# Attention, MoE and gated layer in one kernel: fixed turns of the experts, tile 0's tokens from a short list of its own, high parts first, layer two's lists behind expert 1's weights

## Chip and metric

The kernel runs as one program on one core of a Trainium2 chip. The metric is the device time of one execution in microseconds (us); lower is better. The profile is one such execution, recorded by the hardware profiler. Engines: TensorE (PE; PEld is its weight load), VectorE (DVE), ScalarE (ACT), GpSimd (POOL), SyncE (SP), which here only issues DMAs.

## What is computed

Three stages follow each other. Inputs are float32: q, k, v of shape 2x8x768x64, 16 centroids for each head, 8 experts of 512x1024 and 1024x512, and three matrices of a last layer with 1536 columns.

```python
mask = q_assign[:, :, :, None] == k_assign[:, :, None, :]      # nearest centroid of each query and key
scores = np.where(mask, scale * q @ k.T, -1e9)
attn_out = softmax(scores) @ v                                   # -> x: 1536 tokens x 512

logits = x @ w_gate                                              # 8 experts
expert_idx = np.argmax(logits, axis=1)
for e in range(E):
    mask = expert_idx == e
    out[mask] = gate_w[mask, None] * (np.maximum(x[mask] @ w1[e], 0.0) @ w2[e])

result = ((out @ w_a) * (out @ w_b)) @ w_out
```

For the inputs used, the experts have 198, 119, 169, 188, 162, 192, 206 and 302 tokens, which is 2, 1, 2, 2, 2, 2, 2 and 3 tiles of 128 rows.

## The kernel before

The order of work on each engine is written out by hand; engines wait for each other by semaphores alone (`wait_ge`). On VectorE `link` makes a step wait for the one before it.

**Attention.** 16 heads (`G`), in pairs, six query tiles each. The last step of a head scales its rows of x (`scale_x`, L948) and its share of the gate logits; SP stores the rows to `x_rows` in DRAM (`store_rows`, L444), and POOL adds the logits (`add_logits`, L567), for the last head too. Beside it POOL splits expert 0's weights.

**Weights.** A product of float32 values is made of high and low parts: high x high, high x low and low x high (`product3`, L1291 to L1293, in this order for each slice of the contraction). The weights of an expert are 8 chunks of 128x1024 (`HELD`), 4 for `w1` and 4 for `w2` (`C1`). SP loads chunk `i` into one of 4 stage buffers once chunk `i - 4` is converted (`load_chunk`, L453); POOL converts expert 0's and VectorE all others: `make_high` (L368, a cast) and `make_low` (L372, a subtraction, which raises `s_cv`). Two experts' weights fit in `w_split`. So an expert's chunks overwrite those of the expert two turns earlier, once that expert's last tile is through (`s_hid` for `w1`, `s_yps` for `w2`).

**Routing** (L990 to L1079). From the logits VectorE makes a one-hot of each token's expert (`e_hot`); TensorE multiplies it by a triangle and by ones for each token's rank within its expert, then for the experts' counts, and raises `s_rank` after both. VectorE finds the first tile of each expert (`e_start`), each token's slot, and one-hots of slot row (`row_hot`, one compare of 128x1536) and slot tile. TensorE multiplies them to turn the list round: which token is in each slot (`token_i`, L1032, raises `s_token`). POOL gathers the rows of tiles 0 and 1 by this list (`gather_x`, L620). VectorE then gives a turn to each expert that has tokens (`turn_i`, `turn_start_i`, `turn_expert_i`, raising `s_turns`, L1050), and SP waits for that before it loads the second turn's weights (L506). The last layer's lists (`c_start` to `place_values`, L1056 to L1079) follow at once: 128-row tiles of tokens sorted by expert, without padding. Only then come the conversions of turn 1 (`for r in range(1, E)`).

**Tiles.** `TILES` = 19 tiles of 128 slots. For each, TensorE transposes the gathered rows (`transpose_x`, L1304), makes the hidden layer in two halves of 12 matmuls (`hidden`), transposes it (`transpose_h`, L1328) and makes the output in two halves of 12 matmuls (`expert_out`). `tile(j)` interleaves tile `j` with the hidden halves of tile `j + 1`. ScalarE copies each transposed tile twice, as high part and raw, and POOL subtracts one from the other for the low part (`xT_low` L633, `hT_low` L639). `hidden` of a tile waits for 4 chunks of its expert in `s_cv` and for both parts of x. Where nothing useful is to be done, TensorE multiplies the identity by itself (`spin`, L1144). `find_places` (L1346) is 12 small matmuls for the last layer's lists and stands behind tile 0.

**Last layer.** 36 units of 36 matmuls and their outputs, untouched here.

## Time and profile before

| | |
|---|---|
| median of 3 runs | 841.16 us (841.05 to 843.97) |
| the profiled execution | 842.13 us, its span 839.5 us |
| mean granted TensorE clock | 0.991 |
| PE busy | 814.5 us (97%) |
| DVE busy | 460.5 us (55%) |
| ACT busy | 352.4 us (42%) |
| POOL busy | 363.5 us (43%) |
| DMA | 86.67 MB, mean 103 GB/s |

The profiled execution's time is 2.6 us more than its span, which is the time around it. The chain that ended last lies on PE for 84% of the span, on DVE for 7% and on POOL for 4%. A busy PE counts stand-in matmuls too, and matmuls overlap a little, so that their summed durations say less than the distance of their starts. In a timeline a row gives the start in us, the duration in us, the engine, the line, the operation, what it writes and reads, and in square brackets how long the engine was idle before it and what it waited for.

### The profile page before, as it was taken

What the parts mean: (1) busy time and instruction counts of PE and PEld (TensorE: products, weight loads), DVE (VectorE), ACT (ScalarE), POOL (GpSimd) and SP (SyncE); (2) the same over time, 40 slices, a digit from 0 to 9 for tenths busy, and PEclk for the clock granted to TensorE, in tenths of its full rate; (3) what the DMA queues carried; (4) which work ended last, traced back from release to release, by engine and by line L of the source; (5) the groups of instructions that cost most, each with busy time, mean ns of one, the idle gap of its engine ahead of it and who ended that gap; (6) DMA issues with size and microseconds to landing.
All of it is one profiled execution on the core that took longest, in us unless ns stands there. A gap on an engine that the chain in (4) does not pass through costs nothing.

```text
span 839.5 us, 13318 instructions
## 1 busy us (share of the span) xinstructions
PE 814.5 (97%) x4402; PEld 682.1 (81%) x4403; DVE 460.5 (55%) x705; ACT 352.4 (42%) x711; POOL 363.5 (43%) x295
## 2 busy tenths in 40 slices
PE   8999999999999898999999999999999999999995
PEld 4888898898898487888888888788888888888884
DVE  2879879879886899997777401642121112111110
ACT  1867778778786142434334444211212122121111
POOL 6998988988983344464446454000001000010001
PEclk8999999999999999999999999999999999999998
DMA  7454444454320368776668511500001000010001
GB/s 184 123 124 120 127 129 120 120 132 122 78 84 19 112 223 267 230 263 208 215 204 269 159 38 51 159 16 13 26 13 50 1 13 13 0 51 1 1 0 50
DMA packets 50137, 86.67 MB, mean 103 GB/s; under 512 B 19312, under 2 KB 21360, under 8 KB 50096
## 3 DMA queue, kind: packets, MB, share of 16 engines
q1 hardware_dynamic: 43920, 69.88, 28.6%
q0 software_dynamic: 3440, 11.27, 4.3%
q10 hardware_dynamic: 2736, 4.98, 1.6%
q8 instruction: 25, 0.41, 0.2%
q14 instruction: 16, 0.13, 0.0%
HBM read 73.27 MB, written 11.27 MB: 101 GB/s over the span
## 4 chain that ended last, share of the span: by engine, by line
PE 84%; DVE 7%; POOL 4%; issue 2%; DMA 1%; SPq 0%; ACT 0%; DVEq 0%; POOLq 0%
PE bank L1291 19%; PE bank L1293 19%; PE bank L1292 19%; PE bank L1199 6%; PE bank L1215 4%; PE bank L1183 3%; PE bank L1189 3%; PE bank L1217 3%; DVE w_split L372 2%; PE bank L1228 2%; PE bank L1328 2%; PE bank L1163 2%; DVE w_split L368 2%; PE bank L1214 1%; PE bank L1304 1%
## 5 line engine op out<-in xcount | busy, mean ns | idle before, releaser
L1130 DVE TENSOR_TENSOR ab_raw<-bank,a_sb 128x512 f32<-128x512 f32 x36 | 24.9, 691 | 191.4 <-PE bank L1293 191.4
L958 DVE TENSOR_REDUCE neg_max<-bank 128x1 f32<-128x768 f32 x96 | 91.7, 955 | 37.9 <-PE bank L1189 37.2
L368 DVE CAST w_split<-stage 128x1024 fp32r<-128x1024 f32 x72 | 66.8, 927 | 74.9 <-PE bank L1293 74.4
L372 DVE TENSOR_TENSOR w_split<-stage,w_split 128x1024 fp32r<-128x1024 f32 x72 | 104.6, 1452 | 2.5
L718 ACT ACTIVATE pT_hi<-bank 128x384 fp32r<-128x384 f32 x192 | 84.9, 490 | 46.3 <-PE bank L1199 45.0
L929 DVE TENSOR_TENSOR pT_lo<-bank,pT_hi 128x384 fp32r<-128x384 f32 x192 | 97.5, 550 | 4.5 <-ACT pT_hi L718 4.5
L639 POOL TENSOR_TENSOR hT_lo<-hT_raw,hT_hi 128x512 fp32r<-128x512 f32 x38 | 56.0, 1473 | 89.4 <-ACT hT_raw L777 89.2
L739 ACT ACTIVATE probs<-bank,neg_max 128x768 f32<-128x768 f32 x96 | 87.1, 907 | 11.3 <-DVE neg_max L958 11.3
L1199 PE MATMUL bank<-ident,probs 128*128 128x128 f32 x576 | 81.0, 275 | 1.8 <-ACT probs L739 1.1
L837 ACT ACTIVATE a_sb<-bank 128x512 f32<-128x512 f32 x36 | 21.5, 598 | 136.1 <-PE bank L1293 136.1
L1293 PE MATMUL bank<-x2T_a,w_split 128*128 128x512 f32 x192 | 74.7, 389 | 0.0
L1291 PE MATMUL bank<-x2T_a,w_split 128*128 128x512 f32 x192 | 74.7, 389 | 0.0
L1292 PE MATMUL bank<-x2T_a,w_split 128*128 128x512 f32 x192 | 74.7, 389 | 0.0
L1199 PEld LDWEIGHTS bank<-ident,probs 128*128 128x128 f32 x576 | 65.8, 140 | 10.4 <-DVE pT_lo L929 2.5
L650 POOL DMA_INDIRECT x<-sorted_y,back_i x12 | 11.7, 978 | 129.8 <-PE bank L1340 128.6
L1291 PE MATMUL bank<-w_split,xT_hi 128*128 x152 | 61.7, 406 | 3.5 <-DVE w_split L372 2.6
L1291 PE MATMUL bank<-w_split,hT_hi 128*128 x152 | 63.0, 414 | 0.5 <-issue 0.5
L1215 PE MATMUL bank<-pT_lo,v_split 128*64 128x384 f32 x192 | 61.6, 348 | 0.0
L1293 PE MATMUL bank<-w_split,xT_lo 128*128 x152 | 60.3, 396 | 0.0
L1292 PE MATMUL bank<-w_split,xT_hi 128*128 x152 | 59.9, 394 | 0.0
L1293 PE MATMUL bank<-w_split,hT_lo 128*128 x152 | 59.6, 392 | 0.0
L1292 PE MATMUL bank<-w_split,hT_hi 128*128 x152 | 59.5, 391 | 0.0
(224 smaller groups left out, 1826.0 us busy)
## 6 DMA issues: line engine op xcount, KB each, us to landing
stage<-w SPq DMA_DIRECT2D x64, 512.0 KB, 4.2
q_raw<-qT SPq DMA_DIRECT2D x32, 192.0 KB, 3.7
k_raw<-kT SPq DMA_DIRECT2D x32, 192.0 KB, 3.9
sorted_y<-y_sb ACTq DMA_DIRECT2D x19, 256.0 KB, 4.0
q_pair<-qT SPq DMA_DIRECT2D x8, 384.0 KB, 4.3
k_pair<-kT SPq DMA_DIRECT2D x8, 384.0 KB, 4.9
v_raw<-v_keys SPq DMA_DIRECT2D x16, 192.0 KB, 4.2
stage<-w_a SPq DMA_DIRECT2D x6, 512.0 KB, 4.4
```

What stands on the lines that cost most here:

```text
L368: eng.tensor_copy(dst[:, 0], src).then_inc(s_cvh, 1)
L372: eng.tensor_tensor(dst[:, 1], stage[:, i % STAGES], dst[:, 0].bitcast(F32), ALU.subtract).then_inc(s_cv, 1)
L639: pool.tensor_tensor(hT_lo[:, cols], hT_raw[:, cols], hT_hi[:, cols].bitcast(F32), ALU.subtract).then_inc(s_hl, 1)
L718: act.activation(pT_hi[:, half, part * GT:(part + 1) * GT, j * P:(j + 1) * P], pT_ps[part].rearrange("p (k q) -> p k q", q=P), ACT.Copy).t ...
L739: act.activation(probs[:, qt % 2], scores[qt % 2][:, 0:S], ACT.Exp, bias=neg_max[:, qt % 2:qt % 2 + 1], accum_out=row_sum[:, slot, qt, 0:1 ...
L929: dve.tensor_tensor(pT_lo[dst], pT_ps[part].rearrange("p (k q) -> p k q", q=P), pT_hi[dst].bitcast(F32), ALU.subtract).then_inc(s_pl, 1)
L958: dve.tensor_reduce(neg_max[:, qt % 2:qt % 2 + 1], scores[qt % 2][:, 0:S], AX_X, ALU.max, negate=True).then_inc(s_max, 1)
L1199: last = pe.transpose(pT_ps[part][:, j * P:(j + 1) * P], probs[:, slot, kt * P:(kt + 1) * P], ident[:, :])
L1215: pe.matmul(oT_ps[0:D], v_split[:, slot, kt, 0], pT_lo[:, half, kt], start=False, stop=False)
L1291: pe.matmul(ps, lh, rh, start=first, stop=False)
L1292: pe.matmul(ps, lh, rl, start=False, stop=False)
L1293: return pe.matmul(ps, ll, rh, start=False, stop=last)
```

## The change

1. *Fixed turns.* Each expert has at least one tile: the thresholds that count its tiles begin at -1 (`tile_thr`), and expert `e` has turn `e`. The turn lists go; SP no longer waits for them or reads them. It issues expert 1's first four loads between the last stores of attention and all others behind them.
2. *Tile 0's own short list.* The rank counts from 1. `first_key` is the rank of expert 0's tokens and 0 for all others; 12 compares of 128x128 make its one-hots (`lane_hot`, used again later), and 12 small matmuls give the tokens of tile 0 alone (`first_i`). POOL gathers tile 0 by it and the other tiles by `token_i`. The counts have a PSUM bank and a semaphore of their own, so that this chain waits only for the ranks. `find_slots` moves behind tile 0's first hidden half.
3. *One-hots in pieces.* `row_hot` and the later `lane_hot` are 12 compares of 128x128 against a per-partition scalar in place of one of 128x1536. The row of an expert's first slot comes straight out of one sum.
4. *Logits.* VectorE adds the last head's share itself, and the difference for the softmax comes behind `e_hot`. The gate's sum and reciprocal come behind `token_i`.
5. *High parts first.* In `hidden` and `expert_out` the 8 matmuls with the high part of the left side come first; the wait for the low part stands before the last 4.
6. *Tile 0 and 1 in another order.* Only tile 0 is transposed before the first hidden half; both of its halves are transposed, then comes its output, and tile 1 behind that.
7. *Layer two's lists* stand behind the 8 conversions of expert 1, ahead of expert 2's; `find_places` stands behind tile 1.

The core of the diff (constants of POOL, ScalarE's matching order and semaphores are left out):

```diff
@@ SP @@
-            for c in range(PAIRS - 1, HELD):
-                load_first(c)
+            load_first(HELD - 1)
             store_head(G - 3, 1)
+            load_expert(HELD)
+            load_expert(HELD + 1)
             store_head(G - 2, 0)
+            load_expert(HELD + 2)
+            load_expert(HELD + 3)
             store_rows(G - 1, 1, 0, GT, 2 * G - 1)
             store_rows(G - 1, 1, GT, QT, 2 * G)
-            sp.wait_ge(s_turns, 1)
-            for r in range(1, E):
-                e = sp.value_load(turn_expert_i[0:1, r:r + 1], min_val=0, max_val=E - 1)
...
+            for i in range(HELD + 4, EXPERT_CHUNKS):
+                load_expert(i)
@@ POOL @@
+                token = first_i[:, 0:1] if j == 0 else token_i[:, j:j + 1]
...
-            pool.wait_ge(s_token, 1)
+            pool.wait_ge(s_first, 1)
             gather_x(0, 0)
-            gather_x(1, 1)
...
             xT_low(0, 0)
+            pool.wait_ge(s_token, 1)
+            gather_x(1, 1)
             gather_x(2, 0)
+            hT_low(0, 0)
+            hT_low(0, 1)
             xT_low(1, 1)
             gather_x(3, 1)
-            hT_low(0, 0)
@@ VectorE @@
+            dve.wait_ge(s_rank, 1)
+            link(dve.tensor_tensor(first_key[:, :], rank[:, :, 0], e_hot[:, :, 0], ALU.mult))
+            for t in range(T):
+                dve.tensor_scalar(lane_hot[:, t, :], row_no[:, 0, :], first_key[:, t:t + 1], -1.0,
+                                  ALU.subtract, ALU.is_equal).then_inc(s_fhot, 1)
+            dve.wait_ge(s_counts, 1)
+            link(dve.tensor_tensor(r_et, counts.unsqueeze(2).to_broadcast([P, E, T]), tile_thr[:, :, :], ALU.is_gt))
+            link(dve.tensor_copy(counts_f[:, :], counts))
+            dve.wait_ge(s_firstT, 1)
+            link(dve.tensor_scalar(first_f[:, :], first_token[:, 0:1], float(P), None, ALU.mult))
+            dve.tensor_tensor(first_i[:, :], first_token[:, 1:2], first_f[:, :], ALU.add).then_inc(s_first, 1)
...
+            for t in range(T):
+                dve.tensor_scalar(row_hot[:, t, :], row_no[:, 0, :], slot_lane[:, t:t + 1], None, ALU.is_equal).then_inc(s_thot, 1)
...
+                if r == 1:
+                    make_place_one_hots()
@@ TensorE @@
+            last.then_inc(s_counts, 1)
             for t in range(T):
-                last = pe.matmul(slot_token, row_hot[:, t, :], tile_tokens[:, t], start=(t == 0), stop=(t == T - 1))
-            last.then_inc(s_slotT, 1)
-            spin(20)
+                pe.wait_ge(s_fhot, t + 1)
+                last = pe.matmul(first_token, lane_hot[:, t, :], packed[:, t, 0:2], start=(t == 0), stop=(t == T - 1))
+            last.then_inc(s_firstT, 1)
+            spin(19)
...
+                for c in range(C1):
+                    for part in range(2):
+                        pe.matmul(h_ps[half], xT_hi[:, par, cols(c)], ring((r % 2) * HELD + c, part)[:, cols(half, 512)],
+                                  start=(c == 0 and part == 0), stop=False)
+                if half == 0:
                     pe.wait_ge(s_xl, j + 1)
...
-            pe.wait_ge(s_turns, 1)
             transpose_x(0, 0)
             spin(3)
-            transpose_x(1, 1)
-            spin(3)
-            r_first = turn_of(0)
-            hidden(0, 0, 0, r_first)
-            hidden(0, 0, 1, r_first)
+            hidden(0, 0, 0, 0)
+            find_slots()
+            hidden(0, 0, 1, 0)
             transpose_h(0, 0)
+            transpose_h(0, 1)
+            pe.wait_ge(s_tiles, 1)
...
+                if static(j) and j == 0:
+                    expert_out(0, 0, 0)
+                    transpose_x(1, 1)
+                    expert_out(0, 1, 0)
+                    r_next = expert_of(1)
+                    hidden(1, 1, 0, r_next)
+                    transpose_x(2, 0)
+                    hidden(1, 1, 1, r_next)
+                    transpose_h(1, 0)
+                    return
...
-                if static(j) and j == 0:
+                if static(j) and j == 1:
                     find_places()
```

What that does to the order of instructions shows best on two engines. On VectorE, around the first conversions, the order before is this (`place_hot` and `packed` belong to layer two's lists, L368 and L372 convert a chunk):

```order
L1047 CAST turn_start_i<-turn_start_f 128x8
L1050 CAST turn_expert_i<-turn_expert_f 128x8
L1056 TENSOR_TENSOR r_tmp<-bank,before_e 128x64
...
L1064 TENSOR_TENSOR lane_hot<-row_no,place_lane 128x1536
L1066 TENSOR_TENSOR place_hot<-tile_row,place_tile 128x144
...
L1079 TENSOR_TENSOR place_values<-place_hot,packed 128x1008
L368 CAST w_split<-stage 128x1024
L372 TENSOR_TENSOR w_split<-stage,w_split 128x1024
L368 CAST w_split<-stage 128x1024
```

And this is it in the changed kernel, from the gate's reciprocal to the first conversion of expert 2 (L372 and L376 convert a chunk there; the dots stand for six more of the eight chunks and for the lists' middle):

```order
L1067 TENSOR_TENSOR token_i<-bank,token_f 128x19
L1071 RECIPROCAL gate<-l_sum 128x12
L372 CAST w_split<-stage 128x1024
L376 TENSOR_TENSOR w_split<-stage,w_split 128x1024
...
L1076 TENSOR_TENSOR r_tmp<-counts_f,before_e 128x64
...
L1088 TENSOR_SCALAR lane_hot<-row_no,place_lane_f 128x128 x12
...
L1096 TENSOR_TENSOR place_values<-place_hot,packed 128x1008
L1105 TENSOR_LOAD e_start_i
...
L372 CAST w_split<-stage 128x1024
L376 TENSOR_TENSOR w_split<-stage,w_split 128x1024
```

The lists stood ahead of all conversions and now stand between expert 1's eight and expert 2's.

On TensorE, from the counts to the first tile, before:

```order
L1279 MATMUL bank<-e_hot,ones 128x8 x12
L1144 MATMUL bank<-ident_bf 128x512 x23
L1284 MATMUL bank<-tile_tokens,row_hot 128x38 x12
L1144 MATMUL bank<-ident_bf 128x512 x20
L1304 MATMUL bank<-ident,x_in 128x128 x4
L1144 MATMUL bank<-ident_bf 128x512 x3
L1304 MATMUL bank<-ident,x_in 128x128 x4
L1144 MATMUL bank<-ident_bf 128x512 x3
```

And in the changed kernel, where L1302 is tile 0's short list and L1309 is `find_slots`:

```order
L1298 MATMUL bank<-e_hot,ones 128x8 x12
L1302 MATMUL bank<-packed,lane_hot 128x2 x12
L1162 MATMUL bank<-ident_bf 128x512 x19
L1327 MATMUL bank<-ident,x_in 128x128 x4
L1162 MATMUL bank<-ident_bf 128x512 x3
L1342 MATMUL bank<-w_split,xT_hi 128x512 x8
L1347 MATMUL bank<-w_split,xT_lo 128x512 x4
L1309 MATMUL bank<-tile_tokens,row_hot 128x38 x12
L1342 MATMUL bank<-w_split,xT_hi 128x512 x8
L1347 MATMUL bank<-w_split,xT_lo 128x512 x4
L1354 MATMUL bank<-ident,h_relu 128x128 x8
```

The 12 small matmuls on all slots moved from before the first transposes to behind the first 12 hidden matmuls, and 27 of the 49 stand-in matmuls are gone.

## Rows read from the trace of the kernel before

**Rows 1.** The page: busy time of the engines; one kind of DMA issue.

```profile
PE 814.5 (97%) x4402; PEld 682.1 (81%) x4403; DVE 460.5 (55%) x705; ACT 352.4 (42%) x711; POOL 363.5 (43%) x295
...
stage<-w SPq DMA_DIRECT2D x64, 512.0 KB, 4.2
```

**Rows 2.** Windows: length; busy us of PE, PEld, DVE, ACT, POOL; PEclk, DMA, GB/s.

```profile
272.50:291.20 18.70, 15.30 (x104) 7.20 (x102) 15.92 (x53) 2.30 (x5) 4.54 (x5) 1.00 0.26 83
291.20:322.60 31.40, 31.40 (x160) 25.54 (x160) 30.85 (x32) 11.51 (x22) 18.14 (x12) 1.00 0.73 241
...
330.20:830.00 499.80, 497.74 (x2306) 411.50 (x2305) 190.51 (x206) 143.13 (x255) 112.85 (x87) 1.00 0.27 87
```

**Rows 3.** Timeline of TensorE before tile 3.

```profile
309.54 0.63 PE L1346 MATMUL bank<-place_values,lane_hot 128*128 128x84 bf16 x12
...
322.24 0.39 PE L1293 MATMUL bank<-w_split,hT_lo 128*128 x1
...
325.19 0.49 PE L1291 MATMUL bank<-w_split,xT_hi 128*128 x1 [2.56 <-DVE w_split L372]
```

**Rows 4.** Timeline of VectorE's conversions, and one POOL row beside them.

```profile
294.92 0.69 DVE L368 CAST w_split<-stage 128x1024 fp32r<-128x1024 f32 x1
...
298.58 1.30 POOL L639 TENSOR_TENSOR hT_lo<-hT_raw,hT_hi 128x512 fp32r<-128x512 f32 x1 [4.20 <-ACT hT_raw L777]
...
298.64 1.79 DVE L368 CAST w_split<-stage 128x1024 fp32r<-128x1024 f32 x1
...
312.10 0.69 DVE L368 CAST w_split<-stage 128x1024 fp32r<-128x1024 f32 x1
...
313.96 0.69 DVE L368 CAST w_split<-stage 128x1024 fp32r<-128x1024 f32 x1
...
323.55 1.23 DVE L372 TENSOR_TENSOR w_split<-stage,w_split 128x1024 fp32r<-128x1024 f32 x1
```

**Rows 5.** Timeline of the routing and of tile 0's start, several engines.

```profile
273.30 0.25 DVE L999 TENSOR_REDUCE l_max<-logits 128x12 f32<-128x96 f32 x1 [0.40 <-POOL logits L567]
...
275.39 0.44 PE L1279 MATMUL bank<-e_hot,ones 128*128 128x8 bf16 x12
...
275.94 0.26 DVE L1013 TENSOR_TENSOR r_tmp<-bank,tile_thr 128x96 f32<-128x96 f32 x1 [0.42 <-PE bank L1279]
...
282.25 0.18 DVE L1032 TENSOR_TENSOR token_i<-bank,token_f 128x19 int32<-128x19 f32 x1
...
287.04 0.63 PE L1304 MATMUL bank<-ident,x_in 128*128 128x128 f32 x4 [0.71 <-DMA x_in<-x_rows,token_i]
...
288.88 1.96 POOL L633 TENSOR_TENSOR xT_lo<-xT_raw,xT_hi 128x512 fp32r<-128x512 f32 x1 [3.15 <-ACT xT_raw L767]
```

**Rows 6.** Timeline of VectorE: small instructions that follow each other.

```profile
332.15 0.16 DVE L1098 TENSOR_SCALAR scaled<-bank 128x12 f32<-128x12 f32 x1
332.23 0.16 DVE L1099 TENSOR_SCALAR scaled<-bank 128x12 f32<-128x12 f32 x1
```

**Rows 7.** Timeline of TensorE in the second pair of heads.

```profile
47.41 0.61 PE L1183 MATMUL bank<-k_hl,q_hh 128*128 128x512 f32 x2 [1.25 <-POOL k_hl L548]
```

**Rows 8.** Timeline of VectorE: the lists for layer two.

```profile
286.06 0.23 DVE L1056 TENSOR_TENSOR r_tmp<-bank,before_e 128x64 f32<-128x64 f32 x1
...
287.95 1.75 DVE L1064 TENSOR_TENSOR lane_hot<-row_no,place_lane 128x1536 bf16<-128x1536 bf16 x1
...
289.74 1.26 DVE L1066 TENSOR_TENSOR place_hot<-tile_row,place_tile 128x144 f32<-128x144 f32 x1
...
291.71 1.61 DVE L1076 CAST packed<-gate_rest 128x12 bf16<-128x12 f32 x1
```

**Rows 9.** Windows of TensorE alone: length, busy us (count), PEclk, DMA, GB/s.

```profile
326.20:329.50 3.30, 3.30 (x10) 0.52 0.85 286
8.70:15.30 6.60, 6.60 (x26) 0.52 1.01 191
```

More of the change, by code:

```diff
@@ L338, in attention_moe_gate @@
         UNITS = 3 * FB
[L339 removed]
+        Y_TILES = [min(TILES, ((4 * g + 4) * P - 1 + (E - 1) * P) // P + 1) for g in range(3)]
         EARLY = Y_TILES[0] + 1
@@ L979, in pair @@
                 head(pp, 1)
+            dve.memset(first_f[:, :], 0.0).then_inc(s_hid, 1)
+            dve.memset(first_key[:, :], 0.0).then_inc(s_yps, 1)
             dve.memset(row_sum[:, :, :, 1:2], 1e-9).then_inc(s_line, 1)
@@ L997, in _ @@
             r_tiles = r_tmp[:, 0:TILES * (E - 1)].rearrange("p (j e) -> p j e", e=E - 1)
-            dve.wait_ge(s_logit, G)
+            one_t = lambda m: m[:, :].unsqueeze(2)
+            one_value = lambda i: packed[:, :, i:i + 1]
+            last_b = slice((B - 1) * QT, B * QT)
+            dve.wait_ge(s_logit, G - 1)
+            dve.wait_ge(s_x, 2 * G)
+            link(dve.tensor_tensor(logits[:, last_b, :], logits[:, last_b, :], x_head[:, (G - 1) % 2, :, D:XW], ALU.add))
             link(dve.tensor_reduce(l_max[:, :], logits[:, :, :], AX_X, ALU.max))
-            dve.tensor_tensor(l_dif[:, :, :], logits[:, :, :], by_t(l_max[:, :]), ALU.subtract).then_inc(s_gx, 1)
             link(dve.tensor_tensor(l_eq[:, :, :], logits[:, :, :], by_t(l_max[:, :]), ALU.is_equal))
@@ L1005, in _ @@
+            link(dve.tensor_reduce(tile_e_f[:, :], r_tiles, AX_X, ALU.add))
+            dve.tensor_copy(tile_e_i[:, :], tile_e_f[:, :]).then_inc(s_tiles, 1)
+            dve.wait_ge(s_slotT, 1)
+            link(dve.tensor_scalar(token_f[:, :], slot_token[:, 0], float(P), None, ALU.mult))
+            dve.tensor_tensor(token_i[:, :], slot_token[:, 1], token_f[:, :], ALU.add).then_inc(s_token, 1)
             dve.wait_ge(s_ge, 1)
@@ L1275, in _, with find_slots @@
             for t in range(T - 1):
-                pe.matmul(rank[:, t + 1:T, :], ones[:, :], e_hot[:, t:t + 1, :].to_broadcast([P, T - 1 - t, E]),
-                          start=False, stop=(t == T - 2))
+                last = pe.matmul(rank[:, t + 1:T, :], ones[:, :], e_hot[:, t:t + 1, :].to_broadcast([P, T - 1 - t, E]),
+                                 start=False, stop=(t == T - 2))
+            last.then_inc(s_rank, 1)
             for t in range(T):
                 last = pe.matmul(counts, ones[:, :], e_hot[:, t, :], start=(t == 0), stop=(t == T - 1))
-            last.then_inc(s_rank, 1)
-            spin(23)
-            pe.wait_ge(s_thot, 3)
+            last.then_inc(s_counts, 1)
             for t in range(T):
-                last = pe.matmul(slot_token, row_hot[:, t, :], tile_tokens[:, t], start=(t == 0), stop=(t == T - 1))
-            last.then_inc(s_slotT, 1)
-            spin(20)
+                pe.wait_ge(s_fhot, t + 1)
+                last = pe.matmul(first_token, lane_hot[:, t, :], packed[:, t, 0:2], start=(t == 0), stop=(t == T - 1))
+            last.then_inc(s_firstT, 1)
+            spin(19)
+            def find_slots():
+                pe.wait_ge(s_thot, T + 2)
+                for t in range(T):
+                    last = pe.matmul(slot_token, row_hot[:, t, :], tile_tokens[:, t], start=(t == 0), stop=(t == T - 1))
+                last.then_inc(s_slotT, 1)
             def product3(ps, left, right, first, last):
```

217 lines of the change are left out of this document (101 added, 116 removed).

## The prediction

> **What bounds the kernel now.** I read the page first: TensorE is busy 97% of the span, no other engine more than 55% [rows 1]. So time can only come from TensorE's gaps, its stand-in matmuls on the identity (`spin`), or its clock. The windows by stage show where these lie [rows 2]: after attention (until 272.5 us) 18.7 us of routing with few useful matmuls, 31.4 us without a gap, then a gap and a slow stretch, and from 330.2 on 499.8 us with 497.7 busy at full clock. The change touches the routing, the first two tiles and the gap. The rest can gain nothing: its matmuls, their number and their shapes stay.
>
> The gap has one releaser: the first hidden matmul at 325.19 waits for VectorE's `w_split` (L372) [rows 3]. In the order of TensorE it is tile 3, the first of expert 2. It waits for `s_cv` at 20, the 20th chunk converted; 8 of these are expert 0's, so VectorE must convert 12 chunks after the routing. It starts them at 294.92 and ends the twelfth at 323.55 + 1.23 = 324.78; TensorE follows 0.41 later [rows 3, 4]. VectorE never waits in that stretch (30.85 of 31.4 us busy [rows 2]), so not the weights' DMA but VectorE itself is the limit. **The end of the kernel therefore hangs on when VectorE has done its twelfth chunk, and not on when TensorE starts tile 0.** A chunk takes 1.86 us where nothing disturbs it (CASTs at 312.10 and 313.96 [rows 4]). Twelve are 22.3; from 294.92 to 324.78 are 29.9. The missing 7.5 us are seven stretched instructions, one for each of the seven POOL subtractions in the stretch; the first pair stands at 298.58 and 298.64, a CAST of 1.79 for 0.69 [rows 4]. That is 1.08 us each.
>
> **The first tile's tokens.** First the ends of the chain, then what comes between. The last logits addition moves from POOL to VectorE, where `l_max` waits 0.40 for it [rows 5]; the addition takes most of that itself: 0.1 us saved. `l_dif` leaves the path to `e_hot`: 0.2, what such an instruction of 96 elements takes (0.26 [rows 5]) less its overlap. `first_key` waits for the ranks and no longer for the 12 count matmuls: 0.3 (0.44 from the first start to the last end [rows 5]). So it starts at 275.94 - 0.6 = 275.3 and takes 0.2. Then come 12 compares of 128x128. No such row exists. Independent instructions of 12 elements start 0.08 apart (332.15, 332.23 [rows 6]); a CAST of 1024 takes 0.69 [rows 4] against 0.16 for 12 [rows 6], 0.52 ns an element, which makes 0.15 for 128. Bounds 1.0 and 1.8 us for 12; I take the middle, 1.4. The compare and copy of the counts (0.29 + 0.2) and the two instructions that make `first_i` (0.4) end at 277.8. Today `token_i` ends at 282.25 + 0.18 = 282.43 [rows 5]: **the gather of tile 0 starts 4.6 us earlier**, and its transposes at 287.04 - 4.6 = 282.4 [rows 5]. SP's last stores of `x_rows` are issued when they are today, right after the last x_head; no row shows them late, and I take them as landed.
>
> The VectorE: DVE Perf Modes page of the Trainium skill (section on the TRN2 errata: SBUF-source operations) puts such a bf16 compare from SBUF at 58 + 128/4 cycles, 0.09 us, so 12 at 1.1 us. That is an estimate from the page, inside my bounds; it would take 0.3 from this term and 0.3 from the lists below.
>
> **Tile 0 on TensorE.** High parts first: the first eight matmuls start when `xT_hi` is there, some 1.4 after the transposes, and end at 285.6. The subtraction of the low part starts 1.84 after the transposes, as at 288.88, and takes 1.3 as at 298.58 [rows 4, 5]: ready at 285.8 with the hop between engines. Four more matmuls at 0.23 (322.24 to the end at 322.47 [rows 3]) and the 12 small ones of `find_slots` (some 0.4, as the 12 of the counts [rows 5]) end at 287.3. The second half, the transposes, the output and tile 1's hidden halves follow with small gaps (for the relu, 0.6, and for `hT_lo`), since nothing is interleaved now. I add 60 matmuls at 0.227, five groups of transposes at 0.36 and for the gaps 1.3: the state that today is reached at 309.54, where `find_places` starts [rows 3], is reached at 304.0. With a tile and `find_places`, 12.9 us (309.54 to 322.47), TensorE stands before tile 3 at 316.9, **5.6 us earlier than today**.
>
> **VectorE, the path that counts.** `find_slots` now stands behind tile 0's first hidden half, so VectorE, done with its own routing at about 283.3 (17 chained instructions of 0.2 to 0.4 and 12 compares, 5.5 us, behind 277.8), waits until 287.3 for it. `token_f`, `token_i` and the three instructions of the gate follow, with their chain 1.0 us: 288.3. POOL gets a memset, two small iotas and a select more, and `turn_no`'s iota less, ahead of the k_hl for which TensorE waits 1.25 us at 47.41 [rows 7]. I put that at 0.2 us (0 to 0.5), and it shifts everything. VectorE starts chunk 8 at 288.5 instead of 294.92: 6.4 earlier. Its data is there, since four loads are issued before the end of attention. Each later load has the conversion of three other chunks, 5.6 us, to land in, and takes 4.2 [rows 1].
>
> But the lists for layer two no longer lie ahead of these chunks. They lie between the eighth and the ninth, and tile 3 needs twelve: they are still on the path, only in another place of it. Today they last from 286.06 to 294.92 [rows 4, 8], 8.86 us. Two of them are stretched by POOL, 1.26 for about 0.3 and 1.61 for 0.2 [rows 8]: 6.5 without. The one compare of 1.75 becomes 12 (1.4), one small cast is added (0.2), two fillings of `packed` go (0.2): 6.1. POOL's subtractions in the stretch are eight: the two halves of tile 0, x and both halves of tile 1, x of tiles 2 and 3, and the first half of tile 2. The sum: 288.5 + 22.3 + 6.1 + 8 x 1.08 = 325.5, and TensorE 0.4 later, **325.9 against 325.19: +0.7**. What TensorE gained turns into a gap of 9.0 us in place of 2.6.
>
> Here a rule speaks against the change. The stretched rows show that a POOL subtraction costs VectorE 1.08 us [rows 4]. The SBUF — State Buffer page of the Trainium skill (section "SBUF: two separate sides") says that the pair of ports which both engines share is an exclusive lock for a whole instruction. By it each subtraction would cost up to its own length, 1.3, which is another 1.8 us over eight. The trace agrees with the kind of wait and falls short of that length.
>
> **The clock.** After today's gap the granted clock is full for 1 us and then at 0.52 from 326.2 to 329.5, in the main the 1.2 GHz level [rows 9]: 1.65 us lost. The other stretch at that level lasts 6.6 us, after the thin start of the program [rows 9]: 3.3 lost. I take it that a gap of 9.0 costs no less than today's and no more than that, and choose 2.2, nearer to today's, since only the gap's length differs: +0.5.
>
> **The sum.** 842.13 (the profiled execution) + 0.7 + 0.5 = 843.3. Against the median of the runs, 841.16, that is **842.4 us**. Work costed at nothing: the weight loads (covered by conversions; uncovered, 4 us once), the removed turn instructions (282.35 to 286.06 on VectorE; they fall into the wait for `find_slots` anyway), `find_places` one tile later (in the gap).
>
> **Rivals.**
> 1. *TensorE keeps its lead.* If VectorE were ready by 316.9, the gap and the slow clock would vanish: 5.6 + 2.6 + 1.6 = 9.8 less, 831.4. For it: the first four chunks are loaded early. Against it: VectorE's work up to the twelfth chunk does not fit. It would need the lists off the path and few disturbed instructions; lists at half price (3.0) and half the stretches (4.3) give 7.3, 835, and it would take both. Chance 0.12.
> 2. *The clock falls in tile 0.* Between the last `spin` and the first hidden matmuls lie gaps of some 1.0 and 0.5 us. Today's (0.71 before the transposes [rows 5] and others) leave the clock at 1.00 [rows 2]. If it falls before `find_slots`, 12 matmuls at 0.43 for 0.227 and the transposes make 2.7 us, VectorE waits for them, and the twelfth chunk is late by that; with the full 3.3 at the gap, 842.4 + 2.7 + 1.1 = 846.2, slower by 0.6%. It decides from some nine matmuls at the low level on (1.9 us). Chance 0.10.
> 3. *The change does half of what it says:* POOL disturbs less, since the 24 short compares need few ports or its subtractions meet VectorE waiting. Three stretches fewer and 0.8 for the compares give 838.4. Chance 0.15.
>
> The forecast keeps 0.63.
>
> **How the numbers follow.** Down: 0.8 (compares at 1.0), three stretches (3.2): 838.4. Up: 0.8 (compares at 1.8), 1.8 (the longer stretches), 1.1 (clock): 846.1. The range 838.3 to 846.1 leaves out rival 1 and the end of rival 2. A measurement of this kernel tells 0.5%, 4.2 us, from no change. Faster by more needs less than 837.0: rival 1, 0.12. Slower by more is over 845.4: rival 2 and some of the upper end, 0.10. The rest, 0.78, is no change.
>
> **What would show it.** Right: `first_i` near 277.8; the transposes of tile 0 near 282.4; VectorE's first CAST near 288.5; the twelfth chunk near 325.5; a gap before the first hidden matmul of tile 3 of 7 to 10 us with VectorE as releaser and the clock at half behind it. Wrong: a gap of under 4 us (rival 1), a clock below 1 before 290 us (rival 2), fewer than six stretched instructions (rival 3), or a gap elsewhere, which nothing here foresees.

## The result, and the profile after

The changed kernel takes 846.91 us, the median of 6 runs (846.63 to 848.53), beside 842.5 us for the kernel before on the same chip (841.05 to 844.81): ratio 1.0053, 95% interval 1.0033 to 1.0073. It is slower by 0.5%, 4.5 us above the 842.4 forecast and 0.8 above the range. (The forecast was built on 841.16, the median of the first three of the six times of the kernel before.) The profiled execution took 846.94 us with a span of 845.2.

The page of the changed kernel, for [rows 1]: the engines' busy time, and the loads of weights.

```profile
PE 816.7 (97%) x4387; PEld 685.8 (81%) x4388; DVE 459.2 (54%) x736; ACT 352.8 (42%) x711; POOL 360.6 (43%) x297
...
stage<-w SPq DMA_DIRECT2D x64, 512.0 KB, 4.3
```

This tells no more than that TensorE is still the busy one. The last x_head, with which both kernels enter the part that was changed, is a good mark to divide the span at. It starts at 272.52 before and at 276.00 now, so **3.5 us of the 5.7 by which the span grew lie ahead of the part whose time the prediction added up**, in attention. The windows of TensorE there in the kernel before (stretch, length, busy us, clock, DMA share, GB/s):

```profile
8.00:15.00 7.00, 7.00 (x30) 0.57 1.01 196
15.00:19.50 4.50, 3.88 (x21) 0.92 0.61 193
19.50:35.50 16.00, 14.18 (x97) 1.00 0.54 134
```

And in the changed kernel:

```profile
8.00:15.00 7.00, 5.86 (x44) 1.00 1.03 196
15.00:19.50 4.50, 2.10 (x10) 1.00 0.60 208
19.50:35.50 16.00, 15.91 (x72) 0.57 0.53 132
```

Before, the clock is low from 8 to 15 us, under stand-ins. They take longer, TensorE reaches its wait for POOL's `k_hl` late and idles 0.93 us, and the clock stays full behind it. Now it is full from 8 to 15, the stand-ins end early, TensorE idles 2.49 us, and over the next 16 us the granted clock averages 0.57, under attention's own matmuls: 72 of them in the window instead of 97. The first matmul behind the wait starts at 19.80 before and 19.59 now, so the change to POOL's constants did not move it. Here `k_hl` is what the first scores read; POOL makes it. The row in the timeline of the changed kernel:

```profile
19.59 0.59 PE L1201 MATMUL bank<-k_hl,q_hh 128*128 128x512 f32 x2 [2.49 <-POOL k_hl L554]
```

From x_head on, for [rows 2]: windows of the changed kernel, with the same columns (length; busy us of PE, PEld, DVE, ACT, POOL; PEclk, DMA, GB/s).

```profile
276.00:292.58 16.58, 16.02 (x101) 9.02 (x100) 11.53 (x59) 1.97 (x4) 2.81 (x3) 0.90 0.08 22
292.58:320.76 28.18, 27.93 (x136) 22.25 (x134) 27.49 (x45) 11.65 (x22) 18.23 (x13) 1.00 0.63 206
320.76:335.50 14.74, 6.34 (x27) 4.94 (x27) 14.46 (x17) 0.78 (x2) 0.00 (x0) 0.65 0.58 185
335.50:835.00 499.50, 497.43 (x2305) 411.15 (x2305) 189.60 (x205) 143.05 (x255) 111.13 (x86) 1.00 0.27 87
```

First the routing, then somewhat over two tiles' work without a gap, then a gap and a slow stretch, and the long rest at full clock. The third window is what the forecast called the gap of 9 us; VectorE is busy all through it. The timeline of TensorE there, for [rows 3]:

```profile
319.68 1.08 PE L1417 MATMUL bank<-w_split,hT_lo 128*128 x4
322.10 0.64 PE L1372 MATMUL bank<-place_values,lane_hot 128*128 128x84 bf16 x12 [1.34 <-DVE place_values L1096]
329.80 3.77 PE L1342 MATMUL bank<-w_split,xT_hi 128*128 x8 [7.07 <-DVE w_split L376]
```

TensorE waits 1.34 us for the lists, does `find_places`, and waits 7.07 us for VectorE's twelfth chunk. That makes 9.0 us from 320.76 to tile 3, the length that the forecast gave the gap. Eight matmuls at the low clock then take 3.77. Tile 3 starts 53.80 us after x_head, and 52.67 before. VectorE's timeline of the changed kernel, for [rows 4] and [rows 8]: conversions and lists.

```profile
292.58 0.70 DVE L372 CAST w_split<-stage 128x1024 fp32r<-128x1024 f32 x1
...
296.32 1.79 DVE L372 CAST w_split<-stage 128x1024 fp32r<-128x1024 f32 x1
298.14 2.19 DVE L376 TENSOR_TENSOR w_split<-stage,w_split 128x1024 fp32r<-128x1024 f32 x1
...
306.81 1.78 DVE L372 CAST w_split<-stage 128x1024 fp32r<-128x1024 f32 x1
309.77 1.78 DVE L372 CAST w_split<-stage 128x1024 fp32r<-128x1024 f32 x1
312.73 0.22 DVE L1076 TENSOR_TENSOR r_tmp<-counts_f,before_e 128x64 f32<-128x64 f32 x1
...
313.53 0.71 DVE L1079 TENSOR_TENSOR r_tmp<-r_tmp,e_hot 128x96 f32<-128x96 f32 x1
...
315.49 3.08 DVE L1088 TENSOR_SCALAR lane_hot<-row_no,place_lane_f 128x128 bf16<-128x128 bf16 x12
...
319.30 1.27 DVE L1094 TENSOR_TENSOR gate_rest<-gate_rest,packed 128x12 f32<-128x12 f32 x1
...
320.83 1.21 DVE L1096 TENSOR_TENSOR place_values<-place_hot,packed 128x1008 bf16<-128x1008 bf16 x1
321.96 0.69 DVE L372 CAST w_split<-stage 128x1024 fp32r<-128x1024 f32 x1
```

And the routing, for [rows 5]:

```profile
278.82 0.17 DVE L1034 TENSOR_TENSOR first_key<-bank,e_hot 128x12 f32<-128x12 f32 x1 [0.51 <-PE bank L1294]
279.03 2.04 DVE L1036 TENSOR_SCALAR lane_hot<-row_no,first_key 128x128 bf16<-128x128 bf16 x12
279.34 1.98 PE L1302 MATMUL bank<-packed,lane_hot 128*128 128x2 bf16 x12 [0.25 <-DVE lane_hot L1036]
281.18 5.79 PE L1162 MATMUL bank<-ident_bf 128*128 128x512 bf16 x19
281.67 0.16 DVE L1043 TENSOR_TENSOR first_i<-bank,first_f 128x1 int32<-128x1 f32 x1
286.81 0.60 PE L1327 MATMUL bank<-ident,x_in 128*128 128x128 f32 x4
291.53 0.18 DVE L1066 TENSOR_SCALAR token_f<-bank 128x19 f32<-128x19 f32 x1 [3.58 <-PE bank L1309]
```

The 5.7 us of span are therefore 3.5 ahead of x_head, 1.1 (53.80 - 52.67) from there to tile 3, and 1.1 behind it. The last of these is the clock: it is low until 335.5, which is 5.7 us of work at half speed, 2.8 lost, where 1.65 were lost before [rows 9].

### The profile page after: what moved, and what is told of

Read it like the earlier page. It is cut to its first block, busy times and chain, and to the rows that moved or that the text cites. A ratio compares the mean times of both kernels' runs of the same rounds, so it can differ in the third digit from the quotient of the medians.

```text
span 845.2 us, 13127 instructions
## 1 busy us (share of the span) xinstructions
PE 816.7 (97%) x4387; PEld 685.8 (81%) x4388; DVE 459.2 (54%) x736; ACT 352.8 (42%) x711; POOL 360.6 (43%) x297
## 4 chain that ended last, share of the span: by engine, by line
PE 88%; DVE 7%; issue 2%; POOL 1%; DMA 1%; ACT 0%; SPq 0%; DVEq 0%; POOLq 0%
PE bank L1314 12%; PE bank L1315 12%; PE bank L1316 12%; PE bank L1413 7%; PE bank L1342 7%; PE bank L1217 7%; PE bank L1201 4%; PE bank L1233 4%; PE bank L1207 4%; PE bank L1417 4%; PE bank L1347 4%; PE bank L1235 3%; PE bank L1181 2%; DVE w_split L376 2%; PE bank L1246 2%; PE bank L1354 2%
## 5 line engine op out<-in xcount | busy, mean ns | idle before, releaser
L372 DVE CAST w_split<-stage 128x1024 fp32r<-128x1024 f32 x72 | 65.9, 915 | 76.4 <-PE bank L1347 53.1
L376 DVE TENSOR_TENSOR w_split<-stage,w_split 128x1024 fp32r<-128x1024 f32 x72 | 102.9, 1429 | 2.5
L650 POOL TENSOR_TENSOR hT_lo<-hT_raw,hT_hi 128x512 fp32r<-128x512 f32 x38 | 52.5, 1383 | 92.1 <-ACT hT_raw L793 91.9
L1342 PE MATMUL bank<-w_split,xT_hi 128*128 (+1 forms) x304 | 79.2, 403 | 7.2 <-DVE w_split L376 7.1
L1217 PE MATMUL bank<-ident,probs 128*128 128x128 f32 x576 | 83.0, 279 | 1.2 <-DVE pT_lo L948 1.1
L1413 PE MATMUL bank<-w_split,hT_hi 128*128 (+1 forms) x304 | 79.5, 403 | 0.5 <-issue 0.5
L1217 PEld LDWEIGHTS bank<-ident,probs 128*128 128x128 f32 x576 | 67.6, 143 | 9.7 <-DVE pT_lo L948 2.5
L1342 PEld LDWEIGHTS bank<-w_split,xT_hi 128*128 128x128 f32 x304 | 56.6, 192 | 18.9 <-issue 7.8
L1413 PEld LDWEIGHTS bank<-w_split,hT_hi 128*128 128x128 f32 x304 | 54.3, 188 | 10.8 <-issue 0.7
L787 ACT ACTIVATE h_relu<-bank 128x512 f32<-128x512 f32 x38 | 22.8, 599 | 86.3 <-PE bank L1347 86.3
L1201 PE MATMUL bank<-k_hl,q_hh 128*128 128x512 f32 x192 | 54.4, 365 | 2.5 <-POOL k_hl L554 2.5
```

Source lines behind the costliest of these rows:

```text
L376: eng.tensor_tensor(dst[:, 1], stage[:, i % STAGES], dst[:, 0].bitcast(F32), ALU.subtract).then_inc(s_cv, 1)
L1201: pe.matmul(ps[:, lo:hi], q_hh[:, slot, at], k_hl[:, slot, lo:hi], start=True, stop=False)
L1217: last = pe.transpose(pT_ps[part][:, j * P:(j + 1) * P], probs[:, slot, kt * P:(kt + 1) * P], ident[:, :])
L1342: pe.matmul(h_ps[half], xT_hi[:, par, cols(c)], ring((r % 2) * HELD + c, part)[:, cols(half, 512)], start=(c == 0 and part == 0), stop=False)
L1413: pe.matmul(y_ps, hT_hi[:, cols(k)], ring((r % 2) * HELD + C1 + k // 2, part)[:, cols(k % 2, 512)], start=(k == 0 and part == 0), stop=False)
```

## Experiments

The span of each profiled execution is divided at the start of the last x_head, since the executions differ ahead of it whatever the kernel. "Rest" is the span less x_head. Ratios are against the kernel before on the same chip. The runs stand on three chips besides that of the result: b_again, a_start_spin, a_slots_early and a_lists_late on one; a_again, b_start_spin, b_lists_late and a_both on the second; b_late_spin, a_late_spin and a_both_mixed on the third. Medians of different chips are compared below only beside the rest of the span.

| run | median us | ratio [95%] | span | x_head | rest |
|---|---|---|---|---|---|
| before (first profile) | 841.16 | | 839.5 | 272.52 | 567.0 |
| the change (first profile) | 846.91 | 1.0053 [1.0033, 1.0073] | 845.2 | 276.00 | 569.2 |
| b_again | 842.52 | 0.9992 [0.9965, 1.0020] | 843.1 | 277.69 | 565.4 |
| a_again | 846.19 | 1.0031 [1.0009, 1.0053] | 843.7 | 275.64 | 568.1 |
| a_start_spin | 843.25 | 1.0013 [0.9987, 1.0039] | 841.1 | 272.68 | 568.4 |
| b_start_spin | 841.08 | 0.9976 [0.9957, 0.9995] | 840.7 | 273.77 | 566.9 |
| a_slots_early | 844.22 | 1.0008 [0.9985, 1.0030] | 842.5 | 276.62 | 565.9 |
| a_lists_late | 838.53 | 0.9952 [0.9927, 0.9978] | 838.3 | 276.32 | 562.0 |
| b_lists_late | 838.25 | 0.9940 [0.9916, 0.9963] | 834.5 | 272.27 | 562.2 |
| b_late_spin | 836.44 | 0.9920 [0.9892, 0.9949] | 834.6 | 272.40 | 562.2 |
| a_late_spin | 836.07 | 0.9912 [0.9883, 0.9941] | 834.4 | 273.34 | 561.1 |
| a_both | 831.45 | 0.9873 [0.9838, 0.9907] | 829.5 | 272.38 | 557.1 |
| a_both_mixed | 839.32 | 0.9965 [0.9941, 0.9989] | 836.0 | 272.54 | 563.5 |

On these three chips the kernel before ran 31, 29 and 17 times beside them: medians 843.97, 844.52 and 843.5, and from 839.0 to 847.6 in all.

### The start: does the change do it?

**b_again** is the kernel before, unchanged.

> The kernel before, unchanged, profiled once more. In its profile the clock falls at 8.7 to 15.3 us, under stand-in matmuls, and the last x_head is at 272.5. In the changed kernel's profile it falls at 21.8 to 35.2, under attention's own matmuls, and the last x_head is at 276.0. Theory A (chance of the execution): this run shows either pattern, and its times lie at 841 or at 844 to 845 with a mean clock of 0.99 or 0.98. Theory B (the change causes it): this run shows the early fall again, the last x_head within 0.5 us of 272.5, and all its times but outliers near 841.

Its profile is of an execution in which the clock fell in attention: TensorE idles 3.14 us for `k_hl`, and x_head is at 277.69, later than in the changed kernel. Windows of TensorE in b_again:

```profile
8.00:15.00 7.00, 5.86 (x40) 1.00 1.04 197
15.00:19.50 4.50, 1.51 (x7) 0.90 0.62 206
19.50:35.50 16.00, 15.85 (x63) 0.50 0.50 129
```

So the 3.5 us ahead of x_head need no change to the kernel: the kernel before has such executions too.

**a_start_spin** and **b_start_spin** lengthen the stand-ins ahead of that wait, so that they cover it at either clock.

```diff
             hot_transposes(0)
-            spin(14)
+            spin(26)
```

> The changed kernel with 26 in place of 14 stand-in matmuls before the first scores, so that TensorE does not idle from 17.1 to 19.6 us. Theory (the idle before the first scores makes the clock fall at 21.8): the clock stays at 1.00 from 20 to 40 us, the last x_head is near 272.5 to 273, and the time is 3 to 3.5 us under the changed kernel's, about 843.5. Rival (the fall comes whatever TensorE does there, or the extra POOL and VectorE work delays attention): the last x_head stays at 275 to 276, and the time within 1 us of 846.9.

> The kernel before with 26 in place of 14 stand-in matmuls before the first scores. Theory (TensorE's idle time of 1 to 3 us before the first scores lets the clock fall under attention's own matmuls in some executions of either kernel): no clock below 0.95 from 20 to 40 us in the profile, the last x_head near 272.5, fewer times above 843, and a median 1 to 3 us under that of the kernel before. Rival (the start has nothing to do with it): the same spread and the same median within 0.7 us.

In a_start_spin the clock is 1.00 from 16 to 48 us and x_head stands at 272.68. In no profile with 26 stand-ins does it fall from 20 us on (b_start_spin, b_late_spin, a_late_spin, a_both and a_both_mixed are the others), while it fell in five of the seven with 14: in those five TensorE had idled 2.23 to 3.14 us for `k_hl`, in the two others 0.93 and 0.96. With 26, x_head lies at 272.38 to 273.34 in the four profiles of the changed kernel's code and at 272.40 and 273.77 in the two of the other's, so the change itself moves nothing there that these profiles could show.

The times agree for the kernel before: none of the 11 of b_start_spin is above 842.41, where over half of those with 14 stand-ins are above 843. Two of the ten times of a_start_spin are still 846.7 and 846.9, and no profile shows where these lost their time. The rest of the span is not changed, 568.4 and 566.9. That is 1.5 us between the two kernels; the medians, 843.25 and 841.08, are 2.2 apart.

**a_again**, the changed kernel once more, was for the size of the difference.

> The changed kernel, unchanged, timed with more runs beside the kernel before. Theory (the 3.5 us of attention in the first profile of the change were a fall of the clock that comes in some executions of either kernel; the change itself costs 2 to 3 us between the last x_head and the end): from the last x_head to the end of the span 568 to 569.5 us against 565.4 and 567.0 in the two profiles of before, and a ratio of 1.002 to 1.004. Rival (the change makes the start slower): x_head at 276 or later in the profile, a median of 846.5 to 847 and a ratio of 1.005 or more.

The ratio is 1.0031, again slower. The rest of its span is 568.1. Over the three profiles of each kernel with nothing else edited from x_head on, it is 568.6 with the change (569.2, 568.1, 568.4) and 566.4 without (567.0, 565.4, 566.9): **the change costs 2.1 us, 0.25%**. Of this, 1.0 is tile 3's later start, which hardly varies (53.3 to 54.0 us behind x_head with the change, 52.7 in all three without). The other 1.1 is the low clock behind the gap, which does vary: by the clock windows it costs 2.8, 1.4 and 2.6 us with the change and 1.65, 0 and 1.7 without. In b_again the clock did not fall behind the gap at all, which is why its 565.4 is the lowest.

Whether the change makes the fall at the start likelier stays open. With 14 stand-ins it came in all four profiles of the changed kernel's code and in one of three of the other's. The times lean the same way. Those of the kernel before lie in two groups, with none between 842.3 and 843.4: 39 of 93 are in the lower one. Of the changed kernel's 18, only two (842.4 and 842.7) lie below 844, and none of the six that gave the result. But a time alone doesn't say where the clock fell.

### The lists on VectorE's path

**a_lists_late** puts the lists behind the conversions of expert 4, where VectorE has time, and `find_places` behind tile 10.

```diff
-                if r == 1:
+                if r == 4:
                     make_place_one_hots()
-                if r == 2:
+                if r == 6:
                     dve.wait_ge(s_placeT, 1)
...
-                if static(j) and j == 1:
+                if static(j) and j == 10:
                     find_places()
```

> The changed kernel with layer two's lists behind expert 4's conversions instead of expert 1's, and with find_places behind tile 10. Theory (VectorE's path to the twelfth chunk sets the time): the twelfth chunk ends 8 to 10 us earlier, the gap before tile 3 shrinks from 7.1 to about 1 us, the slow clock behind it goes, and the time falls by 9 to 11 us to 836 to 838. Rival (TensorE's gap moves on to tiles 5 or 7, since VectorE is as late there): gaps of 3 us or more before tile 5 or 7, and a gain of less than 6 us.

Tile 3 in a_lists_late, from TensorE's timeline:

```profile
323.36 2.54 PE L1342 MATMUL bank<-w_split,xT_hi 128*128 x8 [2.84 <-DVE w_split L376]
```

It starts 47.04 us after x_head instead of 53.80, the gap shrinks from 7.07 to 2.84, and 6.6 us of the rest are gone (568.6 to 562.0). That is less than expected (a gap of 1 us, 9 to 11 us of gain). The lists took 9.2 us out of VectorE's way, but POOL's subtractions that had met the lists now meet conversions: eight of these are stretched and not five, which gives some 3 us back. VectorE still releases TensorE, with nothing but conversions in its way.

**b_lists_late** does the same to the kernel before (there the code from `c_start` to `place_values` becomes a function called at `r == 4`, the rest is as above).

> The kernel before with one part changed: layer two's lists behind expert 4's conversions, find_places behind tile 10. VectorE's first CAST then waits for the first chunk's load, issued at 287.4, and comes at 291.5 to 292 instead of 294.92 (for a last x_head at 272.5). Theory (the twelfth chunk sets the time): the gap of 2.6 us before tile 3 and the slow clock behind it go, 3.5 to 4.5 us faster than the kernel before. Rival (the chunks' loads or more stretches take its place): a gap of over 1 us stays and the gain is under 2 us.

Here the gap before tile 3 is gone, and the rest of the span is 562.2, the same as with the change. But VectorE now shows a wait that the lists had hidden. Its timeline in b_lists_late:

```profile
285.62 0.17 DVE L1050 CAST turn_expert_i<-turn_expert_f 128x8 int32<-128x8 f32 x1
290.70 2.27 DVE L368 CAST w_split<-stage 128x1024 fp32r<-128x1024 f32 x1 [4.91 <-DMA stage<-w]
```

The first weights of expert 1 are asked for behind `s_turns`. With the lists in front VectorE never waited for them; without them it waits 4.91 us. In this kernel that costs nothing yet, since the twelfth chunk ends 48.54 us behind x_head and tile 3 starts at 48.95, with TensorE busy until then. But a TensorE that came there earlier would find VectorE no earlier. The early loads of the change remove the wait. That late lists and an earlier tile 0 are worth little without them is argued from these rows; no run leaves the early loads out of the changed kernel.

### find_slots and what the change is worth then

**a_slots_early** puts `find_slots` back ahead of tile 0's hidden half, with the lists where the change has them.

```diff
             transpose_x(0, 0)
-            spin(3)
+            find_slots()
+            spin(1)
             hidden(0, 0, 0, 0)
-            find_slots()
```

> The changed kernel with find_slots right behind tile 0's transposes (in place of two of three stand-in matmuls) instead of behind its first hidden half. Theory (VectorE waits 3.6 us there, on the path): its first CAST comes 3.3 to 3.7 us earlier, the gap before tile 3 shrinks by as much, and the time falls by 3 to 4 us to about 843.3. Rival (the wait is hidden by something else, for example the weights' loads): the twelfth chunk moves by less than 1.5 us, and the time by less than 1.5.

The first CAST stands 13.84 us behind x_head instead of 16.58, and tile 3 at 51.75 instead of 53.80: 2.05 us, less than the 3.3 to 3.7 expected. VectorE's timeline in a_slots_early shows where a part of it went: a small step of the gate, 0.17 in the changed kernel, takes 1.09 beside a POOL subtraction (288.85 to 290.13) that VectorE used to wait through.

```profile
289.07 1.09 DVE L1070 TENSOR_SCALAR l_sum<-l_sum 128x12 f32<-128x12 f32 x1
```

**a_both** is the changed kernel with all three: late lists, early `find_slots`, 26 stand-ins.

> The changed kernel with layer two's lists behind expert 4, find_slots right behind tile 0's transposes, and 26 stand-in matmuls before the first scores. Theory (VectorE's path is all that keeps TensorE's lead from counting): VectorE's twelfth chunk ends about 2 us earlier than in the run with late lists alone, the gap before tile 3 is under 1.5 us, the clock stays full behind it, and the time is 833 to 836. Rival (a gap of the same length stays, since POOL's subtractions then stretch more instructions, or it moves to a later tile): gaps of 2.5 us or more in sum between 290 and 400 us, and 837 to 839.

It takes 831.45 us (831.20 to 832.39), ratio 0.9873 [0.9838, 0.9907], and beats both kernels; 833 to 836 was expected. Its windows from x_head on, with all engines' columns:

```profile
272.40:288.00 15.60, 14.06 (x99) 8.30 (x98) 14.09 (x61) 1.97 (x4) 4.02 (x4) 1.00 0.11 26
288.00:330.00 42.00, 41.75 (x203) 33.82 (x202) 40.96 (x34) 17.19 (x32) 25.44 (x16) 1.00 0.75 251
```

No gap is left before tile 3, which starts 43.81 us behind x_head, and the clock stays at 1.00. TensorE's timeline of a_both:

```profile
316.19 2.11 PE L1342 MATMUL bank<-w_split,xT_hi 128*128 x8
```

VectorE's twelfth chunk ends at 315.88, so that the two engines now arrive there together.

**b_late_spin** and **a_late_spin** tell whose gain that is: the two late edits on the kernel before, and on the changed kernel without the early `find_slots`.

> The kernel before with both edits outside the change: late lists and 26 stand-ins at the start. Beside the changed kernel with the same two and find_slots early (831.5 us) it shows what the change itself is worth once layer two's lists are off VectorE's path. Theory: without the lists the limit is the first tile of the experts, which the change brings some 4 to 5 us earlier, so this run stands 4 to 6 us above 831.5: 835.5 to 837.5, with VectorE waiting some 4.9 us for the first chunk of expert 1 (its loads are issued behind s_turns) and no gap before tile 3. Rival (the change is worth nothing anywhere, and the two edits brought all of it): 831 to 833.

> The changed kernel with late lists and 26 stand-ins at the start, but find_slots where the change has it. From the last x_head on it should be what the run with late lists showed, 562.0 us, after an x_head near 272.8: 834.8 of span, 836.5 in all, with a gap of 2 to 3 us before tile 3 and the clock at half behind it. If it comes out within 1 us of 831.5, the early find_slots brings nothing; if it is at 835 to 838, find_slots early is worth 4 to 6 us once the lists are away, more than the 2.05 us it moved tile 3 with the lists in the way.

By the medians b_late_spin stands 5.0 us above a_both, as expected of a change that is worth something once the lists are away, and its wait for the load is 5.36. But a_late_spin stands 4.6 above it too. The chips differ here; by the rest of the span the distances are 5.1 and 4.0. With only the lists moved, the change is worth 1 us or less (561.1 against 562.2 with 26 stand-ins; 562.0 against 562.2 with 14, where the clock fell behind the changed kernel's gap; in a_late_spin it did not, against what was expected). With `find_slots` early it is worth 5.1 (557.1), and tile 3's start moves by the same: 48.9 us behind x_head in b_late_spin, 47.8 in a_late_spin, 43.8 in a_both. The first CAST is at 18.9, 16.8 and 13.9. TensorE's timeline of a_late_spin shows the gap that is left:

```profile
321.14 2.08 PE L1342 MATMUL bank<-w_split,xT_hi 128*128 x8 [2.88 <-DVE w_split L376]
```

**a_both_mixed** is a_both with part 5 undone, the products in the order of before.

```diff
                     pe.wait_ge(s_xh, j + 1)
+                    pe.wait_ge(s_xl, j + 1)
-                for c in range(C1):
-                    for part in range(2):
-                        pe.matmul(h_ps[half], xT_hi[:, par, cols(c)], ring((r % 2) * HELD + c, part)[:, cols(half, 512)],
-                                  start=(c == 0 and part == 0), stop=False)
-                if half == 0:
-                    pe.wait_ge(s_xl, j + 1)
...
+                for c in range(C1):
+                    last = product3(h_ps[half], (xT_hi[:, par, cols(c)], xT_lo[:, par, cols(c)]),
...
```

> The best version with part 5 of the change undone: the products of hidden and expert_out in the order of before (high x high, high x low, low x high for each slice), the wait for the low part ahead of the first matmul. Theory: high parts first saves only where x or h has just been made and nothing is interleaved, tile 0 and 1: 1 to 2 us on TensorE there, and as TensorE then has no gap before tile 3, all of it would show: 832.5 to 833.5. Rival: the low parts are there anyway in all later tiles and tile 0 is masked by ScalarE's second copy: within 0.5 us of 831.5.

839.32 us, 7.9 above a_both where 1 to 2 were expected. TensorE's timeline has two new waits:

```profile
286.70 0.47 PE L1314 MATMUL bank<-w_split,xT_hi 128*128 128x512 f32 x1 [2.09 <-POOL xT_lo L644]
...
295.83 0.76 PE L1314 MATMUL bank<-w_split,hT_hi 128*128 128x512 f32 x1 [2.06 <-POOL hT_lo L650]
```

These two waits are 4.2 us. The output of tile 0 starts 23.3 us behind x_head instead of 18.8, 4.5 later; some 0.5 of that is the low clock under the 19 stand-ins, which this profile has and a_both's has not. Behind the second wait the clock is low as well: it is 0.50 from 295.8 to 298.4 and full from 299 on, some 1.5 us lost. Together that is 6.0 of the 6.3 by which the rest of the span grew. The profiled execution is one of the faster ones (837.71); the times go up to 843.68, and what the slower ones lose is not shown. So part 5 is worth some 6 us once TensorE is what waits. The other parts were not undone one by one, so it isn't shown which pays most.

## Why the prediction was right or wrong

**The start (not foreseen, +3.5 us).** "It shifts everything" was said of POOL's constants, at 0.2 us; that shift did not come. What came ahead of x_head was the clock in attention. The step that failed is the one that put everything ahead of x_head at the 272.5 us of one profile plus that shift, and the start's spread at nothing: the base of the sum (842.13, and 841.16 for the median) and the range rested on terms behind x_head alone. What the runs showed in its place is an x_head at 272.3 to 277.7 us from one execution to another with 14 stand-ins, 276.0 in the profile of the change. The table of before had its three runs at 841.05, 841.16 and 843.97; 77 further executions of that kernel, beside the experiments, reach from 839.0 to 847.6. A range for the changed kernel ought to have held some 3 us for that. Two of the first three times lay in the lower group, by luck of the draw. The wait for `k_hl` that ended at 19.80 and the low clock from 8.7 to 15.3 [rows 9] stood in the trace; what a full clock there would do to the wait was not asked.

**What bounds the kernel (right).** The end did hang on VectorE's twelfth chunk. TensorE stood waiting before tile 3, 44.8 us behind x_head (320.76 - 276.00), and gained nothing from its lead; 44.4 was the forecast. Moving VectorE's lists moved tile 3 by 6.8 us (a_lists_late).

**The first tile's tokens.** The logits, `l_dif` and the counts gave what was said: `first_key` starts 2.82 us behind x_head (2.8 in the forecast). The 12 compares were put at 1.4 us between bounds of 1.0 and 1.8 and took 2.04, outside the bounds: 0.17 each, not the 0.12 of the middle. `first_i` ends 5.83 behind x_head, not 5.3, and the transposes stand at 10.81, not 9.9, the last 0.4 of it in the stand-ins: where the clock did not fall there they stand at 10.2 to 10.4. The two rows that the price was made from were of other types and shapes, and no row of before showed what a bf16 compare of 128 elements costs. The estimate from the Trainium skill's page VectorE: DVE Perf Modes (section on the TRN2 errata), 0.09 us a compare, is further off still: the trace shows 0.17. The same section adds that its row comes out too short for a single operation, with a measured fixed term of about 150 cycles in place of 58. With that the estimate would be (150 + 32) cycles at 0.96 GHz, 0.19 us, close to the trace.

**VectorE's path.** The wait for `find_slots` came (3.58 us), and the first CAST stands 16.58 us behind x_head, 15.8 without the shift in the forecast. (The forecast's own terms for the end of `find_slots`, 285.8 + 0.9 + 0.4, make 287.1 and not the 287.3 it went on with, so the miss is 1.0 by its terms.) From there to the twelfth chunk are 36.9 us; forecast 37.0. Within it two errors cancel. The stretched instructions are eight, as forecast: five conversions, and in the lists a 0.71, one of the 12 compares that make 3.08, and a 1.27. But the 0.71 is stretched by only 0.45, and some others by 1.0 instead of 1.08: 0.8 less in all. The compares of the lists again cost 0.6 more than said. Tile 3 came 1.1 later than before, against 0.5 forecast without the shift.

The SBUF — State Buffer page of the Trainium skill (section "SBUF: two separate sides") has the shared ports locked for a whole instruction. The stretches (1.79 for 0.69, 2.19 for 1.23) are again 1.0 to 1.1 us beside subtractions that take 1.3 where nothing holds them up, as in [rows 4]: the trace agrees with the kind of wait and not with its length.

**The clock behind the gap.** 2.2 was chosen, 2.8 was measured, inside the bounds of 1.65 and 3.3: +0.6 on this term. In a_again the same gap of 7.07 us cost 1.4, below the bounds. So the length of the gap doesn't set this price alone, as the forecast took it.

**The sum.** Forecast +1.2; measured in the profiled executions +4.8 (842.13 to 846.94). The difference of 3.6 is 3.5 at the start less the 0.2 of the shift, 0.6 on the way to tile 3, 0.6 of the clock, less 0.9 by which the time around the span was shorter (1.7 for 2.6 us). From x_head on, the change costs 2.1 us by the profiles, and with the start in it 0.3% in a_again: either is within the "no change" of the forecast.

**The rivals.** Rival 1 (TensorE keeps its lead, 831.4) did not come by itself, and it named what it would take: lists off the path and less in VectorE's way. a_both has the lists off the path and `find_slots` early, and gives 831.45. That this is the number of the rival is in part luck: its other condition, few disturbed instructions, isn't met (seven conversions up to the twelfth chunk are stretched), and a_both has 26 stand-ins. Rival 2 put the clock's fall in tile 0 before `find_slots`. The clock did fall before 290 us, but under the 19 stand-ins (0.65 from 280 to 283), behind 12 small matmuls that came one by one as the compares ended; it cost 0.4 to 0.6 us and not 2.7. Rival 3 (POOL disturbs less) fell: eight stretches.

## What to carry to other kernels

Work that lies between a producer's units is on the path wherever it stands, as long as the consumer waits for a later unit: count the producer's whole work up to that unit, and move the filler behind the last unit that is short. An edit that brings nothing alone may be worth 5 us once another wait is gone, as this change is with late lists and an early `find_slots`. So it is to be tried again after that, and waits that lie hidden in front of it are to be looked for. And mark a point ahead of the change in both traces before dividing up a difference: what the executions differ by there is not the change's.

## What was not expected of the hardware

- A full clock early went with a slower start. With the clock at 1.00 from 8 to 15 us (after, b_again, a_again) the stand-ins ended early, TensorE idled 2.49 to 3.14 us, and the granted clock averaged 0.50 to 0.57 over 16 us of real work; with 0.57 from 8 to 15 (before) it idled 0.93 and the clock stayed at 1.00. The unchanged code before did either, in its two profiles, and reached x_head 5.2 us apart (272.52 and 277.69).
- A low clock came behind 12 matmuls of a few columns that trickled in over 1.98 us with waits between them. It came in four profiles (19 stand-ins in 5.79 to 5.95 us) and not in four others with the same code at that place (4.26, as in a_start_spin).
- Bf16 compares of 128x128 against a per-partition scalar follow each other every 0.17 us (12 in 2.04), where independent instructions of 12 elements start 0.08 apart [rows 6] and one compare of 128x1536 takes 1.75 in all [rows 8]. Cutting the one into twelve cost 0.3 us.
